# A frequency-domain filter and two gated layers on one core: the layout of the second block transposition

## The chip, the cores and the metric

The kernel runs on one core of a Trainium2 chip. The metric is the device time of one execution in microseconds; the time before is the median of three runs. The engines have short names here: PE is TensorE (matrix products, its weight loads are listed as PEld), DVE is VectorE, ACT is ScalarE, POOL is GpSimd, SP is SyncE, which only issues DMAs.

## The reference

Two sequences of 3008 tokens with 256 channels are filtered in the frequency domain, and the 6016 tokens then pass two layers of width 2048.

```python
X = np.fft.rfft(x, axis=1)                  # x: (2, 3008, 256)
F = (filt_r + 1j * filt_i)[None, :, :]      # (1505, 256)
y = np.fft.irfft(X * F, n=3008, axis=1)
h = y.reshape(6016, 256) @ moe_w_in         # (256, 2048)
g = np.where(h > 0, h, np.exp(np.minimum(h, 0)) - 1)
x1 = g @ moe_w_out                          # (2048, 256)
h = x1 @ moe2_w_in
g = h * np.clip(h + 3, 0, 6) / 6
out = g @ moe2_w_out
```

## The kernel before

The kernel has two parts. The first, up to about 141 us of the span, is the filter (the transform); the second, the other 1013 us, is the two layers, with matrix products in three passes each (lines 366 to 368 and 377). The change touches only the first part.

The length 3008 is 64 x 47, and each transform is a 47-point and a 64-point one in a row, forward and back, written as matrix products with constant matrices (`mats`). The work is cut into four blocks of 128 channels by one sequence (`ORDER`), and each block into 8 groups of 16 channels (`GD`): 32 rounds `i` in all (`NG`). In a round, PE runs `part_a` (line 309, 47-point forward), DVE's `turn_a` (line 545) transposes the result in blocks of 32 x 32 from PSUM to `spec`, PE runs `part_x` (line 317, 64-point forward), DVE multiplies by the filter in `products` (lines 552 and 554), PE runs `part_r` (lines 325 and 326, 64-point back), and DVE's `turn_r` (line 563) transposes that, again in blocks of 32 x 32, from PSUM to `back`. PE's loop runs `part_a(i + 2)`, `part_x(i + 1)`, `part_r(i)` in round `i`; DVE's runs `turn_a(i + 2)`, `products(i + 1)`, `turn_r(i)`. PSUM banks, `spec`, `prod_r` and `prod_i` are double.

`back` has two halves, one per block, each `[128, 32, 128]` fp32 in the order (time index `j`, channel `d`). Once all 8 groups of a block are in it, the last stage (47-point back) runs as `part_i(n)`, line 334: 7 pieces (`PIECES`) of up to 5 values of `j`. For each `j` the stationary operand is the 128 x 128 slice `back[:, half, j, :]`, 128 consecutive floats in each partition, and the moving operand is the constant `I1`, 94 columns. Every fp32 product is two instructions on PE and two weight loads, so a full piece is 10 loads and 10 matmuls, a block 64 of each, and all four blocks 256. The pieces of a block are spread over the first 7 of the next block's 8 rounds, one at the end of each (`piece_at`); those of the last block come after round 31.

ACT copies each piece to `ystage` (line 436) and SP stores it to `y0` (line 227). SP issues in a fixed order: in round `i` the filter values of round `i + 2` (`load_f`, line 219, three slots), in every second round more of `x` (line 212, four slots), then the store of the piece before. POOL multiplies the filter by a sign (line 616) and, every third round, adds up and rounds one of 8 sets of layer weights (lines 623 to 636); ACT has the rounding to `w_hi` (line 443) ahead of the copy of a piece in the same queue.

At the start PE runs 6 products on zeroed memory of `back` (line 340), for which DVE clears 512 floats per partition (line 565). After the last piece come two small products (line 360) and the first products of the layers (line 366).

Of the kernel before, what the change touches and what calls it, by code (L numbers as in the profile page):

```python
# [12 lines left out]
P = 128  # L13
# [7 lines left out]
Q, J, N2P = 2, 32, 48  # L21
AROWS = Q * N2P
GD = 16
# [3 lines left out]
ICOL = Q * N2  # L27
# [65 lines left out]
def build(nc, x_dev, f_dev, sign_dev, mats_dev, w_dev, out_dev):  # L93
    with ExitStack() as ctx:
        def sem(name):
            return ctx.enter_context(nc.semaphore(name))

        def sbuf(stack, name, shape, dt=F32):
            return stack.enter_context(nc.sbuf_tensor(name, shape, dt))
# [11 lines left out]
        with ExitStack() as fft:  # L111
            mats = sbuf(fft, "mats", [P, len(MATS) * P])
            sign = sbuf(fft, "sign", [P, K2])
            x_ring = sbuf(fft, "x_ring", [P, XSLOTS, 2 * GCOL])
            f_ring = sbuf(fft, "f_ring", [P, FSLOTS, 2, XCOL])
            spec = sbuf(fft, "spec", [P, 2, GCOL])
            prod_r = sbuf(fft, "prod_r", [P, 2, XCOL])
            prod_i = sbuf(fft, "prod_i", [P, 2, XCOL])
            back = sbuf(fft, "back", [P, 2, J, P])
        op_hi.append(sbuf(ctx, "op1_hi", [P, 7, T], F32R))  # L120
        op_lo.append(sbuf(ctx, "op1_lo", [P, 7, T], F32R))
        g_hi = sbuf(ctx, "g_hi", [P, 4, T], F32R)
# [4 lines left out]
        ps = ctx.enter_context(nc.psum_tensor("ps", [P, 8, 512], F32))  # L127

        def f32(ap):
            return ap.bitcast(F32)  # L130

        def mat(name):
            at = MATS.index(name) * P
            return mats[:, at:at + P]

        def ps_i(n):
            return ps[:, n % 2, 0:IJ * ICOL]

        def ps_a(i):
            return ps[:, 2 + i % 2, :]  # L140

        def ps_x(i):
            return ps[:, 4 + i % 2, 0:XCOL]

        def ps_r(i):
            return ps[:, 6 + i % 2, :].rearrange("p (d k) -> p d k", k=K2P)

        def bank(n):
            return ps[:, n, 0:T]
# [11 lines left out]
        zeroed = sem("zeroed")  # L161
        a_done, x_done, r_done, i_done = sem("a_done"), sem("x_done"), sem("r_done"), sem("i_done")
        spec_ready, prod_ready, back_ready = sem("spec_ready"), sem("prod_ready"), sem("back_ready")
# [25 lines left out]
        def piece_at(i):  # L189

            c, n = i // GROUPS - 1, i % GROUPS
            return c * PIECES + n if 0 <= c < len(ORDER) and n < PIECES else None

        def piece_cols(n):

            j0 = n % PIECES * IJ
            return n // PIECES, j0, min(IJ, J - j0)
# [102 lines left out]
        def _(pe):  # L300
# [27 lines left out]
            def part_i(n):  # L328
                pos, j0, nj = piece_cols(n)
                pe.wait_ge(back_ready, GROUPS * (pos + 1))  # L330
                if n >= 2:
                    pe.wait_ge(i_evac, n - 1)
                for j in range(nj):
                    last = pe.matmul(ps_i(n)[:, j * ICOL:j * ICOL + ICOL], back[:, pos % 2, j0 + j, :],
                                     mat("I1")[:, 0:ICOL], start=True, stop=True)
                last.then_inc(i_done, 1)

            pe.wait_ge(zeroed, 1)
            for _ in range(6):
                pe.matmul(ps[:, 0, :], back[:, 0, 0, :], back[:, 0, 0:4, :].rearrange("p j d -> p (j d)"),  # L340
                          start=True, stop=True)
            pe.wait_ge(a_mat_loaded, 16)
            part_a(0)
# [4 lines left out]
            for i in range(NG):  # L348
                if i + 2 < NG:
                    part_a(i + 2)  # L350
                if i + 1 < NG:
                    part_x(i + 1)
                part_r(i)
                n = piece_at(i)
                if n is not None:
                    part_i(n)
            for n in range(NPIECE - PIECES, NPIECE):
                part_i(n)
# [28 lines left out]
            for u in range(NU + 1):  # L387
                v = u - 1
                s, p = u // PAIRS, u % PAIRS
# [149 lines left out]
        @block.vector  # L539
        def _(dve):  # L540
            def turn_a(i):
                dve.wait_ge(a_done, i + 1)
                if i >= 2:
                    dve.wait_ge(x_done, i - 1)
                dve.transpose(spec[:, i % 2, :], ps_a(i)).then_inc(spec_ready, 1)

            def products(i):
                dve.wait_ge(x_done, i + 1)
                if i >= 2:
                    dve.wait_ge(r_done, i - 1)  # L550
                dve.wait_ge(f_loaded[i % FSLOTS], 16 * (i // FSLOTS + 1))
                dve.tensor_tensor(prod_r[:, i % 2, :], ps_x(i), f_ring[:, i % FSLOTS, 0, :], ALU.mult)
                dve.wait_ge(signed, i + 1)
                dve.tensor_tensor(prod_i[:, i % 2, :], ps_x(i), f_ring[:, i % FSLOTS, 1, :],
                                  ALU.mult).then_inc(prod_ready, 1)

            def turn_r(i):
                pos, g = i // GROUPS, i % GROUPS
                dve.wait_ge(r_done, i + 1)
                if pos >= 2 and g == 0:  # L560
                    dve.wait_ge(i_done, PIECES * (pos - 1))
                dst = back[:, pos % 2, :, g * GD:g * GD + GD].rearrange("p j d -> p d j")
                dve.transpose(dst, ps_r(i)).then_inc(back_ready, 1)

            dve.memset(back[:, 0, 0:4, :], 0.0).then_inc(zeroed, 1)
            for b in range(2):
                dve.memset(ps[:, 6 + b, :], 0.0).then_inc(zeroed, 1)
            turn_a(0)
            turn_a(1)
            products(0)  # L570
            for i in range(NG):
                if i + 2 < NG:
                    turn_a(i + 2)
                if i + 1 < NG:
                    products(i + 1)
                turn_r(i)

            def second_act(u, src, ap, clipped, ready, done):
                dve.wait_ge(ready, u + 1)
                if u < NS * PAIRS:  # L580
                    dve.tensor_scalar(ap, ap, 1.0, -1.0, ALU.min, ALU.add).then_inc(clipped, 1)  # L581
                    dve.wait_ge(clipped, u + 1)
                    dve.tensor_tensor(ap, src, ap, ALU.max).then_inc(done, 1)  # L583
                else:
                    dve.scalar_tensor_tensor(ap, ap, 6.0, src, ALU.min, ALU.mult).then_inc(done, 1)  # L585

            def low(tiles):
                return dve.tensor_tensor(g_lo[:, tiles, :], e[:, tiles, :], f32(g_hi[:, tiles, :]), ALU.subtract)  # L588

            for u in range(NU + 1):  # L590
                v = u - 1
                if v >= 0:
                    dve.wait_ge(hipair, v + 1)
                    low(slice(TILE21, TILE22 + 1)).then_inc(lopair, 1)
                    dve.wait_ge(hi12, v + 1)
                    low(TILE12).then_inc(lo12, 1)
                if u == NU:
                    break
                second_act(u, bank(BANK_B), e[:, TILE11, :], clip11, e11_ready, m11_done)
                dve.wait_ge(p5_done, u + 1)  # L600
                dve.wait_ge(s7_done, u + 1)
                dve.tensor_tensor(h2[:, 1, :], bank(BANK_C), s7[:], ALU.add).then_inc(h22_done, 1)  # L602
                dve.wait_ge(p4_done, u + 1)
                dve.tensor_tensor(h2[:, 0, :], bank(BANK_A), s7[:], ALU.add).then_inc(h21_done, 1)  # L604
                dve.wait_ge(hi11, u + 1)
                low(TILE11).then_inc(lo11, 1)
                second_act(u, h2[:], e[:, TILE21:TILE22 + 1, :], clippair, epair_ready, mpair_done)
                second_act(u, bank(BANK_C), e[:, TILE12, :], clip12, e12_ready, m12_done)
# [121 lines left out]
```

## Time and profile before

| | us |
|---|---|
| median of 3 runs | 1158.13 |
| lowest, highest | 1157.18, 1158.26 |
| the profiled execution, its own time | 1156.32 |
| its span, first to last instruction | 1154.5 |
| PE busy | 1128.6 (98% of the span) |
| DVE busy | 851.0 (74%) |
| ACT busy | 697.8 (60%) |
| POOL busy | 305.0 (26%) |

The granted TensorE clock is 0.998 of full speed over the whole span. A profile row names the line, engine and operation of a group of instructions. Matmuls are pipelined, and the ends in their records are modelled: how long one takes in a stream is read from the starts of two groups that follow each other, not from its duration. A row of the timeline merges neighbours of one line (x10 is ten instructions), and the brackets at its end give the idle time ahead of it and what ended that.

### The profile page before, as it was taken

What the parts mean: (1) busy time and instruction counts of PE and PEld (TensorE: products, weight loads), DVE (VectorE), ACT (ScalarE), POOL (GpSimd) and SP (SyncE); (2) the same over time, 40 slices, a digit from 0 to 9 for tenths busy, and PEclk for the clock granted to TensorE, in tenths of its full rate; (3) what the DMA queues carried; (4) which work ended last, traced back from release to release, by engine and by line L of the source; (5) the groups of instructions that cost most, each with busy time, mean ns of one, the idle gap of its engine ahead of it and who ended that gap; (6) DMA issues with size and microseconds to landing.
All of it is one profiled execution on the core that took longest, in us unless ns stands there. A gap on an engine that the chain in (4) does not pass through costs nothing.

```text
span 1154.5 us, 17183 instructions
## 1 busy us (share of the span) xinstructions
PE 1128.6 (98%) x6288; PEld 1069.8 (93%) x6288; DVE 851.0 (74%) x1347; ACT 697.8 (60%) x1293; POOL 305.0 (26%) x260
## 2 busy tenths in 40 slices
PE   9988999999999999999998899999999999999998
PEld 4655689999999999999998899999999999999998
DVE  6755488888888888887889877666766666666665
ACT  0211356666666666667666666666666666666665
POOL 4655523021211112120338742120302121111000
PEclk9999999999999999999999999999999999999999
DMA  8767400000010101000021200000000001010000
GB/s 254 226 212 216 151 24 28 28 28 28 1 55 1 54 1 49 6 27 28 28 82 55 91 1 28 27 28 27 28 28 28 28 9 46 1 55 1 28 1 28
DMA packets 33589, 59.52 MB, mean 52 GB/s; under 512 B 3456, under 2 KB 23552, under 8 KB 33504
## 3 DMA queue, kind: packets, MB, share of 16 engines
q1 hardware_dynamic: 33504, 58.42, 15.9%
q8 instruction: 50, 0.82, 0.3%
q14 instruction: 35, 0.29, 0.1%
HBM read 39.92 MB, written 18.48 MB: 51 GB/s over the span
## 4 chain that ended last, share of the span: by engine, by line
PE 83%; DVE 5%; POOL 4%; DMA 3%; ACT 2%; issue 2%; SPq 0%; ACTq 0%; DVEq 0%
PE ps L377 43%; PE ps L366 13%; PE ps L367 12%; PE ps L368 12%; DMA f_ring<-f_dev 3%; DVE e L583 2%; DVE e L581 1%; DVE g_lo L588 1%; POOL f_ring L616 1%; POOL w_lo L636 1%; POOL w_lo L634 1%; PE ps L340 1%; PE ps L309 1%; ACT w_hi L443 1%; ACT e L466 1%
## 5 line engine op out<-in xcount | busy, mean ns | idle before, releaser
L588 DVE TENSOR_TENSOR g_lo<-e,g_hi 128x376 fp32r<-128x376 f32 (+1 forms) x384 | 286.1, 773 | 113.5 <-ACT g_hi L494 113.1
L366 PE MATMUL ps<-op_hi,w_hi 128*128 128x376 f32 x896 | 300.4, 335 | 1.4 <-DVE h L602 1.4
L367 PE MATMUL ps<-op_hi,w_lo 128*128 128x376 f32 x896 | 299.7, 334 | 0.0
L368 PE MATMUL ps<-op_lo,w_hi 128*128 128x376 f32 x896 | 299.6, 334 | 0.0
L377 PE MATMUL ps<-g_hi,w_hi 128*128 128x376 f32 x1024 | 259.1, 334 | 7.1 <-ACT g_hi L494 7.1
L653 POOL TENSOR_TENSOR op_lo<-xr,op_hi 128x752 fp32r<-128x752 f32 x64 | 103.5, 1618 | 606.0 <-ACT op_hi L451 606.0
L377 PE MATMUL ps<-g_lo,w_hi 128*128 128x376 f32 x1024 | 259.3, 334 | 2.8 <-DVE g_lo L588 2.8
L377 PE MATMUL ps<-g_hi,w_lo 128*128 128x376 f32 x1024 | 259.8, 335 | 0.0
L377 PEld LDWEIGHTS ps<-g_hi,w_hi 128*128 128x128 f32 x1024 | 184.0, 188 | 9.1 <-ACT g_hi L494 9.0
L377 PEld LDWEIGHTS ps<-g_lo,w_hi 128*128 128x128 f32 x1024 | 184.1, 188 | 6.0 <-DVE g_lo L588 6.0
L377 PEld LDWEIGHTS ps<-g_hi,w_lo 128*128 128x128 f32 x1024 | 184.2, 188 | 0.0
L366 PEld LDWEIGHTS ps<-op_hi,w_hi 128*128 128x128 f32 x896 | 168.7, 188 | 4.6 <-DVE h L602 3.7
L367 PEld LDWEIGHTS ps<-op_hi,w_lo 128*128 128x128 f32 x896 | 168.7, 188 | 0.1
L368 PEld LDWEIGHTS ps<-op_lo,w_hi 128*128 128x128 f32 x896 | 168.5, 188 | 0.0
L581 DVE TENSOR_SCALAR e<-e 128x376 f32<-128x376 f32 (+1 forms) x192 | 94.8, 494 | 52.5 <-ACT e L466 52.1
L489 ACT COPY ps<-ps 128x376 f32<-128x376 f32 x128 | 58.9, 460 | 112.3 <-PE ps L368 112.3
L494 ACT CAST g_hi<-e 128x752 fp32r<-128x752 f32 x128 | 105.3, 823 | 16.7 <-DVE e L583 15.3
L518 ACT CAST g_hi<-e 128x376 fp32r<-128x376 f32 x128 | 64.9, 507 | 80.6 <-DVE e L583 53.8
L602 DVE TENSOR_TENSOR h<-ps,s 128x376 f32<-128x376 f32 x128 | 70.2, 549 | 32.6 <-PE ps L368 28.0
L468 ACT ACTIVATE e<-h 128x752 f32<-128x752 f32 x64 | 53.3, 833 | 62.5 <-DVE h L604 62.5
L585 DVE SCALAR_TENSOR_TENSOR e<-e,ps 128x376 f32<-128x376 f32 x128 | 69.3, 541 | 24.9 <-ACT e L468 24.1
L585 DVE SCALAR_TENSOR_TENSOR e<-e,h 128x752 f32<-128x752 f32 x64 | 64.6, 1009 | 20.2 <-ACT e L468 20.0
(50 smaller groups left out, 1216.5 us busy)
## 6 DMA issues: line engine op xcount, KB each, us to landing
f_ring<-f_dev SPq DMA_DIRECT2D x32, 384.0 KB, 4.8
xr<-y SPq DMA_DIRECT2D x64, 188.0 KB, 3.0
w_raw<-w_dev SPq DMA_DIRECT2D x32, 256.0 KB, 3.8
y<-ystage SPq DMA_DIRECT2D x16, 376.0 KB, 2.5
out_dev<-ystage SPq DMA_DIRECT2D x16, 376.0 KB, 2.5
x_ring<-x_dev SPq DMA_DIRECT2D x15, 384.0 KB, 5.7
y<-ystage SPq DMA_DIRECT2D x24, 235.0 KB, 2.7
x_ring<-x_dev SPq DMA_DIRECT2D x2, 192.0 KB, 3.5
```

Of the source, the lines that this page charges most:

```text
L366: pe.matmul(out, w_hi[:, p, cols], hi, start=start, stop=False, skip_group_check=True)
L367: pe.matmul(out, w_lo[:, p, cols], hi, start=False, stop=False, skip_group_check=True)
L368: pe.matmul(out, w_hi[:, p, cols], lo, start=False, stop=True, skip_group_check=True).then_inc(done, 1)
L377: last = pe.matmul(out_bank(o, t), w[:, p, at:at + P], g[:, tile, :], start=first, stop=final, skip_group_check=True)
L489: act.copy(bank(BANK_B), bank(BANK_A)).then_inc(copy1_done, 1)
L494: act.copy(g_hi[:, TILE21:TILE22 + 1, :], e[:, TILE21:TILE22 + 1, :]).then_inc(hipair, 1)
L518: act.copy(g_hi[:, TILE11, :], e[:, TILE11, :]).then_inc(hi11, 1)
L581: dve.tensor_scalar(ap, ap, 1.0, -1.0, ALU.min, ALU.add).then_inc(clipped, 1)
L585: dve.scalar_tensor_tensor(ap, ap, 6.0, src, ALU.min, ALU.mult).then_inc(done, 1)
L588: return dve.tensor_tensor(g_lo[:, tiles, :], e[:, tiles, :], f32(g_hi[:, tiles, :]), ALU.subtract)
L602: dve.tensor_tensor(h2[:, 1, :], bank(BANK_C), s7[:], ALU.add).then_inc(h22_done, 1)
L653: pool.tensor_tensor(op_lo[s % 2][:, lo:hi, :], xr[:, 1 + lo:1 + hi, :], f32(op_hi[s % 2][:, lo:hi, :]), ALU.subtract).then_inc(op_lo_done, 1)
```

## The change

`back` gets the order (channel `d`, time index `j`) instead of (`j`, `d`). The result of `turn_r` is then one run of 512 consecutive floats per partition, as that of `turn_a` is; before, its 32 values of one `d` lay 512 bytes apart. `part_i` reads for each `j` the slice `back[:, half, :, j]`: 128 floats per partition that lie 32 floats, 128 bytes, apart; before, they lay one beside the other. The cleared memory and the products at the start are written for the new order and have the sizes of before: 512 consecutive floats, 128 of which are the stationary operand. No instruction is added, dropped or moved on any engine, and the waits are those of before.

```diff
--- before.py
+++ after.py
@@ -116,7 +116,7 @@
             spec = sbuf(fft, "spec", [P, 2, GCOL])
             prod_r = sbuf(fft, "prod_r", [P, 2, XCOL])
             prod_i = sbuf(fft, "prod_i", [P, 2, XCOL])
-            back = sbuf(fft, "back", [P, 2, J, P])
+            back = sbuf(fft, "back", [P, 2, P, J])
         op_hi.append(sbuf(ctx, "op1_hi", [P, 7, T], F32R))
         op_lo.append(sbuf(ctx, "op1_lo", [P, 7, T], F32R))
         g_hi = sbuf(ctx, "g_hi", [P, 4, T], F32R)
@@ -331,13 +331,14 @@
                 if n >= 2:
                     pe.wait_ge(i_evac, n - 1)
                 for j in range(nj):
-                    last = pe.matmul(ps_i(n)[:, j * ICOL:j * ICOL + ICOL], back[:, pos % 2, j0 + j, :],
+                    last = pe.matmul(ps_i(n)[:, j * ICOL:j * ICOL + ICOL], back[:, pos % 2, :, j0 + j],
                                      mat("I1")[:, 0:ICOL], start=True, stop=True)
                 last.then_inc(i_done, 1)
 
             pe.wait_ge(zeroed, 1)
             for _ in range(6):
-                pe.matmul(ps[:, 0, :], back[:, 0, 0, :], back[:, 0, 0:4, :].rearrange("p j d -> p (j d)"),
+                pe.matmul(ps[:, 0, :], back[:, 0, 0:4, :].rearrange("p d j -> p (d j)"),
+                          back[:, 0, 0:16, :].rearrange("p d j -> p (d j)"),
                           start=True, stop=True)
             pe.wait_ge(a_mat_loaded, 16)
             part_a(0)
@@ -559,10 +560,10 @@
                 dve.wait_ge(r_done, i + 1)
                 if pos >= 2 and g == 0:
                     dve.wait_ge(i_done, PIECES * (pos - 1))
-                dst = back[:, pos % 2, :, g * GD:g * GD + GD].rearrange("p j d -> p d j")
-                dve.transpose(dst, ps_r(i)).then_inc(back_ready, 1)
-
-            dve.memset(back[:, 0, 0:4, :], 0.0).then_inc(zeroed, 1)
+                dst = back[:, pos % 2, g * GD:g * GD + GD, :].rearrange("p d j -> p (d j)")
+                dve.transpose(dst, ps[:, 6 + i % 2, :]).then_inc(back_ready, 1)
+
+            dve.memset(back[:, 0, 0:16, :], 0.0).then_inc(zeroed, 1)
             for b in range(2):
                 dve.memset(ps[:, 6 + b, :], 0.0).then_inc(zeroed, 1)
             turn_a(0)
```

## Rows read from the trace of the kernel before

**Rows 1.** The page, busy time and share of the span by engine, whole kernel
```profile
PE 1128.6 (98%) x6288; PEld 1069.8 (93%) x6288; DVE 851.0 (74%) x1347; ACT 697.8 (60%) x1293; POOL 305.0 (26%) x260
```

**Rows 2.** Groups by line and shape, 0 to 240 us: count | busy, mean ns | idle before
```profile
L563 DVE STREAM_TRANSPOSE back<-ps 128x512 f32<-128x512 f32 x32 | 34.1, 1066 | 5.2 <-PE ps L326 5.2
...
L334 PE MATMUL ps<-mats,back 128*128 128x94 f32 x256 | 32.2, 274 | 4.4 <-ACT ystage L436 3.3 <-DVE back L563 1.1
L334 PEld LDWEIGHTS ps<-mats,back 128*128 128x128 f32 x256 | 32.0, 191 | 11.5 <-issue 4.6 <-DVE back L563 1.8
...
L545 DVE STREAM_TRANSPOSE spec<-ps 128x512 f32<-128x512 f32 x32 | 22.0, 688 | 18.3 <-PE ps L309 18.0
```

**Rows 3.** Timeline, 19 to 25 us, TensorE: start us, us, what, count
```profile
19.29 0.81 PE L325 MATMUL ps<-prod_r,mats 128*128 128x384 f32 x2
...
21.44 0.81 PE L317 MATMUL ps<-spec,mats 128*128 128x384 f32 x2
22.08 0.81 PE L325 MATMUL ps<-prod_r,mats 128*128 128x384 f32 x2
```

**Rows 4.** Timeline, 19 to 25 us, VectorE: in brackets idle before, releaser
```profile
17.98 1.06 DVE L563 STREAM_TRANSPOSE back<-ps 128x512 f32<-128x512 f32 x1 [0.27 <-PE ps L326]
18.91 0.66 DVE L545 STREAM_TRANSPOSE spec<-ps 128x512 f32<-128x512 f32 x1
...
20.78 1.07 DVE L563 STREAM_TRANSPOSE back<-ps 128x512 f32<-128x512 f32 x1 [0.27 <-PE ps L326]
```

**Rows 5.** Timeline, 31 to 57 us, TensorE, rounds with a piece of the last stage
```profile
36.07 0.81 PE L325 MATMUL ps<-prod_r,mats 128*128 128x384 f32 x2
...
39.98 0.81 PE L325 MATMUL ps<-prod_r,mats 128*128 128x384 f32 x2
...
49.09 1.25 PE L334 MATMUL ps<-mats,back 128*128 128x94 f32 x10
50.18 1.05 PE L309 MATMUL ps<-x_ring,mats 96*128 96x512 f32 x2
```

**Rows 6.** Line 334 by stretches: busy us (instructions) of PE and PEld, clock, DMA
```profile
36.00:65.00 29.00, 8.07 (x64) 8.25 (x64) 1.00 0.61 199
65.00:120.00 55.00, 13.22 (x104) 13.18 (x104) 1.00 0.72 226
120.00:132.00 12.00, 3.08 (x24) 3.15 (x24) 1.00 0.32 103
```

**Rows 7.** TensorE by stretches: busy us (instructions), granted clock, DMA
```profile
36.00:66.00 30.00, 30.00 (x131) 1.00 0.62 202
66.00:120.00 54.00, 46.06 (x197) 1.00 0.71 226
```

**Rows 8.** Timeline, 57 to 132 us, TensorE: first products' matmuls of four rounds
```profile
65.58 0.81 PE L325 MATMUL ps<-prod_r,mats 128*128 128x384 f32 x2
...
71.29 0.91 PE L325 MATMUL ps<-prod_r,mats 128*128 128x384 f32 x2 [1.64 <-DVE prod_i L554]
...
121.23 0.81 PE L325 MATMUL ps<-prod_r,mats 128*128 128x384 f32 x2
...
129.90 0.84 PE L325 MATMUL ps<-prod_r,mats 128*128 128x384 f32 x2
```

**Rows 9.** Chain that ended last, 50 to 70 us: start us, us, what
```profile
51.05 4.36 DMA f_ring<-f_dev
...
63.79 0.77 ACT ystage L436 x2
...
64.73 4.86 DMA f_ring<-f_dev
```

**Rows 10.** Chain that ended last, 128 to 143 us
```profile
131.42 1.05 DVE back L563
...
132.52 1.37 PE ps L334 x10
...
139.89 0.65 PE ps L334 x4
140.54 1.29 PE ps L360 x4
```

## The prediction

> **What bounds the kernel now.** The page comes first: PE is busy for 98% of the span, DVE for 74% [rows 1]. The diff touches only the first 141 us of 1154.5, so the whole span says little, and the groups of that stretch come next [rows 2]. Two facts stand there. The second block transposition (line 563) takes 1066 ns, the first one (line 545) 688 ns, for the same 128 x 512 from PSUM to SBUF. The last stage (line 334) has 256 weight loads.
>
> Then the timeline, to see who waits. In rounds without a piece of the last stage PE starts line 325 every 2.79 us [rows 3], with its groups one straight behind the other: 0.64 us for two matmuls of 384 columns, 0.84 ns a column. DVE waits 0.27 us for PE before each second transposition [rows 4]. So here PE sets the pace, but barely. In rounds with a full piece the round is 3.91 us, from line 325 to line 325 [rows 5]. The 10 matmuls of a piece take 1.09 us up to the next line's start, 109 ns each [rows 5]. By columns, 94 x 0.84 ns would be 79 ns. What spaces them is therefore more likely the weight load: 128 columns in 109 ns, 0.85 ns each, the rate of the moving operand.
>
> From 36 to 66 us PE is busy for 30.00 of 30.00 us. From 66 to 120 us it is busy for 46.06 of 54 [rows 7]. The chain that ended last shows what holds it there: the filter values are requested at 51.05 and again at 64.73 us, and between the two lie their landing, POOL's sums and roundings and the copy of two pieces by ACT at 63.79 [rows 9]. That loop takes 13.7 us for three rounds and holds no transposition. After 120 us PE sets the pace again. At the end of the part the last second transposition (131.42) releases the last block's 64 loads, which run from 132.52 until the next line's products start at 140.54 [rows 10].
>
> **The change part by part.** *The second transposition, 32 times.* It now writes 512 consecutive floats, exactly what the first does. In the steady rounds that is 0.66 us in place of 1.07 [rows 4], so 0.41 us less, 13 us of DVE in all. Nearly all of it lies beside PE's work: in the rounds up to 66 us PE is back to back and DVE waits for it, so DVE only waits longer; from 66 to 120 us DVE waits for DMA and POOL. It is exposed once, at 131.42 us, where the last piece waits for it: **-0.4 us**.
>
> *The strided weight loads, 256 times.* The trace has no stationary operand with a stride, so the price is bounded. Below zero is excluded: 128 columns are still loaded, now at 0.85 ns each. Zero is the lower end, and a weak row speaks for it: line 317 reads 24 of every 32 floats and takes 0.64 us [rows 3], as line 325 does, which reads consecutive ones. But its breaks come every 24 floats, not at every float. The nearest row for a break at each float is the transposition: 0.41 us for 512 elements is 0.80 ns an element. It is a write by another engine, at 512 bytes, but of the same memory and at a step beyond which no two elements lie together. For 128 elements that makes 102 ns more. I take **0.102 us a load**, so 0.211 in place of 0.109. As the upper end I take twice this, since a read may have to wait for its data where a write does not.
>
> [rows 4] show that a stride in this memory costs about what an element costs. The Trainium skill, Advanced Engine Details and Errata, SBUF Cachelines, says that full speed wants accesses that hit the same 16-byte line, and that a different line at each access has a penalty; at 128 bytes each float has its own line. It states no size of the penalty; by it the price is above zero.
>
> What lies on the path, stretch by stretch, with the loads counted in [rows 6]:
>
> - Up to the round that starts line 325 at 65.58 us: 64 loads, PE back to back. 64 x 0.102 = 6.5 us, all exposed. That round now starts at 72.1.
> - From 65.58 to 121.23 us [rows 8] there are 12 rounds and 104 loads in 55.65 us. PE alone would need 12 x 2.80 + 104 x 0.109 = 44.9, so it holds 10.7 us of waits, such as the 1.64 us at 71.29. The windows show 7.9 us of them idle; the rest is in the modelled ends and in loads that wait. With dear loads PE alone needs 33.6 + 104 x 0.211 = 55.5 us, the length that the stretch has already. The 10.6 us added disappear in the waits, and the lag stays 6.5 - 0.1 = 6.4. This holds only if POOL's and SP's loop isn't itself pushed back. It needs the copy of a piece at 63.79 [rows 9]. That is PE's sixth piece, two rounds of 3.91 us behind the one at 49.09 [rows 5]: it ends at 58.0 us now, and 60 dear loads later (6.1 us) at 64.1. So the loop is pushed by 0.3 us there, and further on it has more room.
> - From 121.23 to 129.90 us [rows 8]: 24 loads and no waits to speak of. 24 x 0.102 = 2.4 us. Lag at the last round: 8.8.
> - The last block: 8.0 us now for 64 loads [rows 10], of which 64 x 0.109 = 7.0 are loads and 1.0 is a wait for `ystage`. It becomes 64 x 0.211 = 13.5; the stores then have time. +5.5 us.
>
> *The cleared memory and the first six products*: same sizes, consecutive; 0. *The layers*: untouched, they start later; 0. The instruction order is that of before.
>
> Sum: 8.8 + 5.5 - 0.4 = **+13.9 us**. The profiled execution took 1156.3, so 1170.2. The median of the runs lies 1.8 above it (1158.1): **1172.0**.
>
> **The rivals.**
>
> *B: the stride is free for a load.* Mechanism: PE asks for one float of each partition only every 0.85 ns, and what the transposition shows is a cost of writing, or of DVE's access, not of the memory. For it speaks line 317. Against it speaks that nothing in that row breaks at each float. Then only the -0.4 is left: 1155.9 for the profiled one, **1157.7** for the median. This is the case on the other side of slower, and the point that decides is the price of a load: the waits from 66 to 120 us take up to 10.7 us over 192 loads (0.056 us each), and a price of 0.056 would leave 0.0 at the last round, 64 x 0.056 - 1.0 = 2.6 at the end, minus 0.4: 2.2 us, or 0.2%. Below about 165 ns a load the change can't be told from none; at 211 it is slower.
>
> [rows 5] show 109 ns for a load of 128 consecutive columns. The Trainium skill, TensorE: Matmul & The Clock Gate, LDWEIGHTS, gives the time of a load as the number of columns by 1.2 GHz, 107 ns, and has no term for a stride; the trace agrees for consecutive columns. By this rule the outcome is B.
>
> *C: faster by over 0.2%.* DVE's 13 us would have to count. Place: from 66 to 120 us, where DVE runs late rounds after a DMA wait, the second transposition stands ahead of the next first one in its queue. If it were last there in six rounds, free loads and 0.41 us each would give 0.4 + 2.5: **1155.2**. Against it: the chain of that stretch holds no line 563, and DVE's waits there end with DMA and POOL.
>
> *D: a load pays much more.* At 0.204 us over, twice the price: 64 x 0.204 = 13.1; then 33.6 + 104 x 0.313 = 66.2 against 55.65, +10.5; 24 x 0.204 = 4.9; the end 64 x 0.313 - 8.0 = 12.0; minus 0.4. That is +40.1: **1198**. It decides as soon as the loads take more than all waits can hold, which is at 0.103 each.
>
> **How the numbers follow.** A, the forecast, gets 0.55, with a range of its own from 1166 (0.07 us a load) to 1178 (PE's waits only half used). B gets 0.32, from 1156 to 1159.5, and holds the prices too small to be seen. C gets 0.05, D 0.08. About 0.2%, 2.3 us, is what a measurement of this kernel can tell from no change. A range that leaves out no more than 2 in 10 must hold A and B: 1156.0 to 1178.0, 0.87 with both whole. Faster 0.05, same 0.32, slower 0.63 (A and D).
>
> **What would show it.** Second transposition: the line's mean falls from 1066 to about 688 ns, and DVE's wait for line 326 grows from 0.27 to about 0.6 us in the first rounds; this holds in A and B. The loads: the start of line 309 behind a full piece comes 2.1 us after the start of line 334 in A, 1.09 in B, 3.1 in D. Rounds with a full piece are 4.9 us in A and 3.9 in B. PE's idle time from 66 to 120 us is nearly gone in A. Line 360, behind the last piece, starts near 154.4 us in A and 140.1 in B; from there on both traces are alike. Rounds without a piece stay at 2.79 us in all cases; were they shorter, DVE had been the bound there. The forecast is wrong if the loads in the piece keep 109 ns, if the price lies under 0.056, or if PE's lag pushes the loop of DMA, POOL and ACT so that waits and dear loads add up (then up to 1182).

## The result and the profile after

| | before | changed |
|---|---|---|
| median, us | 1158.2 (4 runs) | 1172.1 (4 runs) |
| lowest, highest, us | 1157.2, 1158.3 | 1171.0, 1172.8 |
| the profiled execution, us | 1156.32 | 1172.80 |
| its span, us | 1154.5 | 1170.9 |

The ratio is 1.012, with a 95% interval from 1.0104 to 1.0136: the change makes the kernel 1.2% slower. The forecast was 1172.0.

Busy time on the page of the changed kernel (its lines after the diff are one higher), to be read beside [rows 1]:

```profile
PE 1155.5 (99%) x6288; PEld 1101.9 (94%) x6288; DVE 843.4 (72%) x1347; ACT 698.8 (60%) x1293; POOL 305.3 (26%) x260
```

DVE lost 7.6 us of work, PE's busy time grew by 26.9. The groups by line and shape, up to 160 us, beside [rows 2] (count | busy, mean ns | idle before):

```profile
L334 PEld LDWEIGHTS ps<-mats,back 128*128 128x128 f32 x256 | 59.2, 309 | 4.8 <-DVE back L564 1.4
L334 PE MATMUL ps<-mats,back 128*128 128x94 f32 x256 | 56.7, 379 | 0.8 <-DVE back L564 0.8
...
L564 DVE STREAM_TRANSPOSE back<-ps 128x512 f32<-128x512 f32 x32 | 22.9, 716 | 9.3 <-PE ps L326 9.3
L546 DVE STREAM_TRANSPOSE spec<-ps 128x512 f32<-128x512 f32 x32 | 22.9, 716 | 49.2 <-PE ps L309 47.6
```

A load of the last stage is on record for 309 ns in place of 191, and both transpositions have the same mean, 716 ns. How long a load really takes is in the starts of the timeline, beside [rows 5, 8]: a piece, then three rounds that answer to 65.58, 121.23 and 129.90 before:

```profile
47.34 2.21 PE L334 MATMUL ps<-mats,back 128*128 128x94 f32 x10
49.39 1.05 PE L309 MATMUL ps<-x_ring,mats 96*128 96x512 f32 x2
...
71.89 0.81 PE L325 MATMUL ps<-prod_r,mats 128*128 128x384 f32 x2
...
126.97 0.81 PE L325 MATMUL ps<-prod_r,mats 128*128 128x384 f32 x2
...
137.87 0.84 PE L325 MATMUL ps<-prod_r,mats 128*128 128x384 f32 x2
```

The piece takes 2.05 us up to the next line, where it took 1.09. The three rounds come 6.31, 5.74 and 7.97 us later than before; 0.23 of it was there already ahead of the first piece (line 325 at 36.30 for 36.07). That is scatter of the start and not the change: in the traces shown here and below, of kernels with either order, the first piece starts anywhere from 36.48 to 37.66 us. A round without a piece still takes 2.79 us, one with a full piece 4.88 in place of 3.91. PE by stretches, beside [rows 7] with 46.06 of 54 us:

```profile
66.00:120.00 54.00, 54.00 (x196) 1.00 0.69 206
```

No wait is left. The end of the part, in the chain that ended last, beside [rows 10]:

```profile
139.40 0.73 DVE back L564
...
140.17 14.29 PE ps L334 x64
154.46 2.57 PE ps L361 x4
...
158.51 0.44 PE ps L367
```

Line 361 (360 before) starts 13.92 us later than before; the forecast of the change in the total was 13.9. But it takes 2.57 us in place of 1.29. The windows of all engines show why: busy us (instructions) of PE, PEld, DVE, ACT, POOL, then the granted clock, DMA share and GB/s:

```profile
142.00:144.00 2.00, 2.00 (x11) 2.00 (x10) 0.00 (x0) 0.55 (x1) 0.00 (x0) 1.00 0.00 0
144.00:146.00 2.00, 2.00 (x11) 2.00 (x10) 0.00 (x0) 0.55 (x1) 0.00 (x0) 0.55 0.32 120
146.00:150.00 4.00, 4.00 (x20) 4.00 (x20) 0.00 (x0) 1.10 (x2) 0.00 (x0) 0.50 0.33 122
...
154.00:156.00 2.00, 2.00 (x6) 1.32 (x5) 0.00 (x0) 0.49 (x2) 0.00 (x0) 0.50 0.47 161
156.00:158.00 2.00, 2.00 (x7) 1.52 (x6) 0.00 (x0) 0.00 (x1) 0.00 (x0) 0.54 0.78 225
158.00:160.00 2.00, 1.95 (x10) 1.32 (x9) 0.00 (x0) 1.55 (x4) 0.05 (x1) 1.00 0.53 168
```

The granted clock falls from 1.00 to 0.50, from 2.4 to 1.2 GHz, within the window from 144 to 146 us, in the last block's 64 dear loads, and is back from 158. Before, it was 1.00 in all of this.

The layers give part of that back, and lose something of their own later. The same instruction of the layers, well behind the filter, first before, then in the changed kernel:

```profile
175.07 0.33 PE L367 MATMUL ps<-op_hi,w_lo 128*128 128x376 f32 x1
189.79 0.33 PE L368 MATMUL ps<-op_hi,w_lo 128*128 128x376 f32 x1
```

It comes 14.72 us later, and that distance holds up to about 610 us. Between 610 and 680 us it grows to 16.49. There the clock fell three times more in the changed kernel's profiled execution, for some 3.4 us each (the windows give 0.53 from 629 to 632.5 us, 0.55 from 649 to 652.5 and 0.53 from 670 to 673.5), and once in that of the kernel before (0.60 from 614 to 618). Other kernels below have none to two such falls in this place, so this part is scatter of single executions.

### The profile page after: what moved, and what is told of

It reads as the page before. It is cut to its first block, busy times and chain, and to the rows that moved or that the text cites. A ratio compares the mean times of both kernels' runs of the same rounds, so it can differ in the third digit from the quotient of the medians.

```text
span 1170.9 us, 17183 instructions
## 1 busy us (share of the span) xinstructions
PE 1155.5 (99%) x6288; PEld 1101.9 (94%) x6288; DVE 843.4 (72%) x1347; ACT 698.8 (60%) x1293; POOL 305.3 (26%) x260
## 4 chain that ended last, share of the span: by engine, by line
PE 94%; DVE 4%; ACT 1%; issue 1%; ACTq 0%
PE ps L378 43%; PE ps L367 13%; PE ps L369 13%; PE ps L368 13%; PE ps L334 5%; PE ps L309 2%; PE ps L317 2%; PE ps L325 2%; PE ps L326 2%; DVE e L584 2%; DVE e L582 1%; PE ps L340 1%; DVE g_lo L589 1%; ACT e L467 1%; PE ps L361 0%
```

## Experiments

The kernel before was measured again beside three groups of the experiments: its medians were 1156.4 us (beside experiment 1 and the steps of 8 and 16 bytes), 1158.8 (experiment 3, the wide operand and 12 bytes) and 1157.7 (the last block, the pairs and 124 bytes), its single runs 1154.5 to 1162.9. A total is therefore compared by ratio and interval with the kernel before of its group, and what is under 2 us is read from the traces.

**1. Which half of the change costs.** The layout of the changed kernel, with consecutive loads:

```diff
-back[:, pos % 2, :, j0 + j],
+back[:, pos % 2, 4 * (j0 + j):4 * (j0 + j) + 4, :].rearrange("p d j -> p (d j)"),
```

> Half of the change alone: the second transposition writes its 512 consecutive floats as in the changed kernel, but each load of the last stage takes 128 consecutive floats of the block, in the old access pattern and so not the right values. Theory (the loads carry all of the loss, DVE's time is hidden): transposition 0.72 us, piece spacing 1.09 us, PE idle from 66 to 120 us as before (7.9 us), and a gain of 0.3 to 0.4 us at the last transposition only, 1157.8. Rival (DVE's 11 us matter in the stretch in which PE waits): waits of line 325 for line 554 shrink, 1155.5 or less. Rival (the loss comes from the transposition colliding with another access when it runs at full speed): 1160 or more.

1157.1 us for 1156.4 before, ratio 1.0004, interval 0.9995 to 1.0014. The group of the second transposition and PE's wait for DVE between 36 and 131 us (total, times, longest):

```profile
L564 DVE STREAM_TRANSPOSE back<-ps 128x512 f32<-128x512 f32 x32 | 22.7, 710 | 4.1 <-PE ps L326 3.9
...
PE ps L325 <- DVE prod_i L555: 6.1, 5, 2.2
```

PE by stretches (busy us, instructions, clock, DMA):

```profile
66.00:120.00 54.00, 46.17 (x191) 0.97 0.75 226
```

The transposition is as quick as in the changed kernel, the kernel is as slow as before, and PE's wait for line 555 did not shrink (6.1 us; 4.7 before over the same stretch; this execution had the clock at 0.50 for some 3 us near 82 us, which the wait may hold in part). DVE's 11 us are hidden, and a quick transposition does no harm by itself. The -0.3 at the last transposition is too small for the interval; the trace has it, as PE's wait of 0.81 us ahead of the last block in place of 1.14.

The other half alone, the layout of before with loads at a step of 128 bytes:

```diff
+flat = back[:, pos % 2].rearrange("p j d -> p (j d)")
-back[:, pos % 2, j0 + j, :],
+flat[:, j0 + j:j0 + j + 4065:32],
```

> The other half alone: the second transposition writes as before, 1.07 us, and each load takes 128 floats of the block that lie 128 bytes apart, as in the changed kernel (other values than the right ones). Theory (the loads carry all of the loss): piece spacing 2.04 us, PE without idle time from 66 to 128 us, half clock at the end of the part, 1172.1 + 0.35 for the slower last transposition = 1172.5. Rival (the loss needs both halves): 1165 or less.

1169.9 us, ratio 1.0117, interval 1.0102 to 1.0133, the changed kernel's 1.012 again. (The 1172.5 expected was counted from a slower sample of the kernel before; the difference to the 1156.4 measured beside it is 13.6 us.) Its groups:

```profile
L335 PEld LDWEIGHTS ps<-mats,back 128*128 128x128 f32 x256 | 59.2, 309 | 5.1 <-DVE back L564 1.8
...
L564 DVE STREAM_TRANSPOSE back<-ps 128x512 f32<-128x512 f32 x32 | 34.9, 1092 | 9.2 <-PE ps L326 9.2
```

309 ns a load, as in the changed kernel, beside a transposition of 1092. PE has no idle time from 66 to 120 us here either, and the clock falls to 0.50 in the last block. The loss is that of the loads alone.

**2. What a load pays for.** The same edit with other steps, one run each (none of these four computes the reference):

> The kernel before with loads of 128 floats that lie 8 bytes apart, two to a 16-byte line (other values than the right ones). Theory 1 (each load element pays when it comes from another 16-byte line than the last, unless two share it): free, piece spacing 1.09 us, about 1158. Theory 2 (any step above one float costs): spacing above 1.3 us, up to 2.04 us and 1172. Theory 3 (cost grows with the distance): 1.1 to 1.2 us.

> The kernel before with loads of 128 floats that lie 16 bytes apart, one to a line (other values than the right ones). Theory 1 (lines of 16 bytes): full price, piece spacing 2.04 us, 1172. Theory 3 (cost grows with the distance, full at 128 bytes): spacing clearly under 2.04 us, 1.2 to 1.5. Theory 4 (only a large power of two costs): free, 1.09 us.

> The kernel before with loads of 128 floats that lie 12 bytes apart (other values than the right ones). Three neighbours in four come from another 16-byte line. If each change of line costs the same, about 0.1 us, unless hidden by the free slot that a second hit gives: three quarters of the price, piece spacing 1.8 us. If the line is fetched in the time of two elements, 128 x 3/4 fetches at 1.6 ns = 154 ns a load: spacing 1.55 us. If only steps of 16 bytes and more cost: 1.15 us.

> The kernel before with loads of 128 floats that lie 124 bytes apart, each in another line, at no power of two (other values than the right ones). Theory (another 16-byte line at each float is all that counts): piece spacing 2.04 to 2.17 us, as at 128 and 16 bytes, 1170 to 1175. Rival (part of the price comes from the distance being a power of two): clearly less, 1.5 us or under.

One piece and the line behind it in each timeline. A step of 8 bytes:

```profile
49.52 1.31 PE L335 MATMUL ps<-mats,back 128*128 128x94 f32 x10
50.66 1.05 PE L309 MATMUL ps<-x_ring,mats 96*128 96x512 f32 x2
```

12 bytes:

```profile
49.92 1.81 PE L335 MATMUL ps<-mats,back 128*128 128x94 f32 x10
51.58 1.05 PE L309 MATMUL ps<-x_ring,mats 96*128 96x512 f32 x2
```

16 bytes:

```profile
47.66 2.34 PE L335 MATMUL ps<-mats,back 128*128 128x94 f32 x10
49.84 1.05 PE L309 MATMUL ps<-x_ring,mats 96*128 96x512 f32 x2
```

124 bytes:

```profile
47.43 2.32 PE L335 MATMUL ps<-mats,back 128*128 128x94 f32 x10
49.58 1.05 PE L309 MATMUL ps<-x_ring,mats 96*128 96x512 f32 x2
```

The last block's pieces follow one another without a round between, so the starts of ACT's copies there show ten whole loads. Before, and at 12 bytes:

```profile
133.91 0.55 ACT L436 COPY ystage<-ps 128x470 f32<-128x470 f32 x1 [3.09 <-PE ps L334]
135.03 0.55 ACT L436 COPY ystage<-ps 128x470 f32<-128x470 f32 x1 [0.56 <-PE ps L334]
```

```profile
143.98 0.55 ACT L437 COPY ystage<-ps 128x470 f32<-128x470 f32 x1 [1.58 <-PE ps L335]
146.12 0.55 ACT L437 COPY ystage<-ps 128x470 f32<-128x470 f32 x1 [1.58 <-PE ps L335]
```

| step, bytes | stretches of 16 bytes (lines) per load | piece between rounds, us | ten loads in the last block, us (clock there) | single run, us |
|---|---|---|---|---|
| 4 (before) | 32 | 1.09 | 1.12 (1.00) | - |
| 8 | 64 | 1.14 | 1.19 (1.00) | 1158.2 |
| 12 | 96 | 1.66 | 2.13 (0.50) | 1167.2 |
| 16 | 128 | 2.18 | 2.33 (0.50) | 1175.1 |
| 124 | 128 | 2.15 | 2.30 (0.50) | 1175.0 |
| 128 (changed) | 128 | 2.05 | 2.18 (0.50) | 1172.1 (median) |

Each piece between rounds is nine such loads and one product of 94 columns (0.08 us): 9 x 0.112 + 0.08 = 1.09 before, 9 x 0.218 + 0.08 = 2.04 at 128 bytes. The first load of the ten is not seen, as it runs beside the product ahead of it.

The distance doesn't count beyond 16 bytes, and a power of two isn't dear (128 bytes is even the cheapest of the last three, for which no run gives a reason). A load of 8 bytes' step is nearly free, one of 12 lies half way. One reading comes near all but that last row: a load takes a line in about 1.8 ns, the time of two of its columns. By it 32 lines are hidden behind the 112 ns of the columns, 64 lines take 115 ns, 96 take 173 and 128 take 230. With nine loads to a piece the measured ones are 118, 176 (1.66 less 0.08, by nine) and 233. It is a fit to these six steps and not shown beyond them. The form of it that stood in the expectation gave 1.55 for 12 bytes, and 1.66 was measured, against 1.8 and 1.15 for the others. The Trainium skill, Advanced Engine Details and Errata, SBUF Cachelines, has the rule that two hits on a 16-byte line absorb the latency and one does not. The runs at 8 and 16 bytes agree.

**3. Where the waits of 66 to 120 us went.** The forecast let 10.7 us of waits swallow the dear loads there. The waits were put down to a loop through ACT, whose copy of a piece stands behind a rounding of weights that waits for POOL. So the copy was moved ahead of it, in the kernel before:

```diff
 for i in range(NG + PIECES):
-    for p in range(PAIRS):
-        if i == w_step(p):
-            weight_hi(p)
     n = piece_at(i - 1) if i <= NG else None
     if n is not None:
         evac_piece(n)
+    for p in range(PAIRS):
+        if i == w_step(p):
+            weight_hi(p)
```

> The kernel before, with ACT copying the piece of the round before ahead of the rounding to w_hi (and not behind it); it computes the whole reference. Theory (the waits of 66 to 120 us come from a loop that runs through ACT's copy standing behind the rounding, so that SP's store and the next request of filter values wait for POOL): the loop is open, PE waits there for at most 2 of 7.9 us, 1148 to 1152 where the kernel before has 1156.4. Rival (POOL's own work, or the DMA engines, set the 13.7 us for three rounds): 1155 to 1157, PE still idle for 6 us or more.

1146.1 us against 1158.8, ratio 0.9888, interval 0.9865 to 0.991. PE from 66 to 120 us, and the chain that ended last in the stretch of [rows 9]:

```profile
66.00:120.00 54.00, 53.89 (x243) 1.00 0.75 231
```

```profile
53.17 1.08 PE ps L334 x10
54.26 0.89 PE ps L309 x2
```

PE is busy for 53.89 of 54 us, and the chain runs on PE, where it ran through DMA and POOL. The cause of the waits is shown, and this kernel is faster than both. It gained more than the 1148 to 1152 us expected: line 360 starts at 130.26 us for 140.38, so 10.1 us were to be had and not only the 7.9 that the windows show idle. The same exchange in the changed kernel:

> The same exchange in the changed kernel; it computes the whole reference. Theory (with dear loads PE sets the pace throughout and has no wait left that the loop causes): nothing, within 0.5 us of the changed kernel, so 13 to 14 us above the kernel before. Rival (the loop still costs the changed kernel something): 2 us or more less than the changed kernel.

1171.6 us (1170.5 to 1172.0), the changed kernel's time; PE from 66 to 120 us:

```profile
66.00:120.00 54.00, 54.00 (x196) 1.00 0.70 205
```

It had no wait to give back. Between these two kernels, both nearly without waits in that stretch, little hides the loads: 1171.6 - 1146.1 = 25.5 us. That is nearly twice the 13.9 of the change itself; the loop's waits had paid for the rest.

**4. The clock.**

> The changed kernel with the constant moving operand of the last stage taken 128 columns wide in place of 94 (the others are zeros, and the next product overwrites them); it computes the whole reference. Theory 1 (the load sets the spacing, and a matmul has 204 ns to fill): piece spacing stays 2.04 us. Theory 2 on the clock (it fell to half in the last block because the loads leave the array idle for 125 of 204 ns, and busier products keep it up): no half clock at 145 to 158 us, line 361 for 1.3 us in place of 2.6, total 2 to 3 us under the changed kernel. Rival on the clock (any row of products spaced by such loads loses it): clock 0.57 from 142 to 158 us as before, no gain.

```diff
-last = pe.matmul(ps_i(n)[:, j * ICOL:j * ICOL + ICOL], back[:, pos % 2, :, j0 + j],
-                 mat("I1")[:, 0:ICOL], start=True, stop=True)
+last = pe.matmul(ps[:, n % 2, j * ICOL:j * ICOL + P], back[:, pos % 2, :, j0 + j],
+                 mat("I1"), start=True, stop=True)
```

1169.9 us (1169.1 to 1171.0), 1.7 under the 1171.6 of the changed kernel with the exchange, measured beside it, and 2.2 under the changed kernel. The single runs overlap (that kernel had 1170.5 to 1172.0), so the trace decides. PE at the end of the part, and the chain there:

```profile
142.00:158.00 16.00, 15.94 (x73) 1.00 0.38 127
```

```profile
139.76 14.34 PE ps L334 x64
154.10 1.27 PE ps L361 x4
```

With 128 columns in the same spacing the clock stays at 1.00, where it was 0.57 over the same window, and line 361 takes 1.27 us. The other traces agree. In all six kernels whose last block has 94 columns and loads at 12 bytes or more (the changed one, with and without the exchange, and the steps of 12, 16, 124 and 128 bytes in the order of before) the clock fell to 0.50 in that row. In none of those with loads at 4 or 8 bytes, nor in this one, did it fall there.

The gain in the total is not all from there. The instruction of the layers that comes at 189.79 us in the changed kernel comes at 189.13 here and at 189.33 in the changed kernel with the exchange, so behind the filter this kernel leads by 0.7 and 0.2 us only. The rest arises between 610 and 680 us, where this profiled execution has no fall of the clock. What half clock in the last block costs a whole run is therefore well under 1 us, not the 2 to 3 expected.

The last block's 64 loads take 14.3 us here too. ACT's copies show the spacing of its pieces, here

```profile
144.46 0.55 ACT L437 COPY ystage<-ps 128x470 f32<-128x470 f32 x1 [1.65 <-PE ps L334]
146.66 0.55 ACT L437 COPY ystage<-ps 128x470 f32<-128x470 f32 x1 [1.65 <-PE ps L334]
```

and in the changed kernel at half clock

```profile
144.90 0.55 ACT L437 COPY ystage<-ps 128x470 f32<-128x470 f32 x1 [1.72 <-PE ps L334]
147.09 0.55 ACT L437 COPY ystage<-ps 128x470 f32<-128x470 f32 x1 [1.64 <-PE ps L334]
```

2.20 and 2.19 us for 10 loads: at a step of 128 bytes half clock doesn't slow the loads, only the products behind them. It does at 12 bytes, where ten loads take 2.13 us at half clock (lines in experiment 2) and 1.76 by the pieces at full clock. The two would fit together if half clock slowed a load's columns only: 213 ns for 128 columns is 1.7 ns each, about twice the 0.85 of before, and the loads at 128 bytes, with 219 ns at full clock, are above that already. This is argued; no run has consecutive loads at half clock to test it.

> The changed kernel, but the last block keeps the old layout and consecutive loads (its values are misplaced). Theory (half clock comes from 64 dear loads in a row with nothing beside them, and the loads cost 0.096 us each): the last block takes 8.0 us again, no half clock, so only the lag of PE up to round 31 is left, 8.0 us: 8 us above the kernel before, 6 under the changed one. Rival (the clock falls for the dear loads of the rounds before, which take 2.04 of every 4.9 us): half clock stays and the gain is 4 us at most.

```diff
+block = back[:, pos % 2, :, j0 + j]
+if pos == len(ORDER) - 1:
+    block = back[:, pos % 2, 4 * (j0 + j):4 * (j0 + j) + 4, :].rearrange("p d j -> p (d j)")
-back[:, pos % 2, :, j0 + j],
+block,
```

with `turn_r` writing the old layout for that block. The expectation errs in one point: writing and reading agree here, and the kernel computes the whole reference. 1164.8 us, ratio 1.0063, interval 1.0047 to 1.008: 7.1 above the kernel before, measured beside it, and 7.3 under the changed kernel. In the trace the products behind the last block start at 148.37 us for 140.38, the 8.0 us expected. PE at the end:

```profile
142.00:158.00 16.00, 15.09 (x97) 1.00 0.44 146
```

No half clock, although the rounds before have the dear loads as ever. In this kernel the fall belongs to the last block's row of them.

**5. A layout between the two,** on top of the exchange of experiment 3:

```diff
-back = sbuf(fft, "back", [P, 2, J, P])
+back = sbuf(fft, "back", [P, 2, J // 2, P, 2])
-back[:, pos % 2, j0 + j, :],
+back[:, pos % 2, (j0 + j) // 2, :, (j0 + j) % 2],
-dst = back[:, pos % 2, :, g * GD:g * GD + GD].rearrange("p j d -> p d j")
-dve.transpose(dst, ps_r(i)).then_inc(back_ready, 1)
+dst = back[:, pos % 2, :, g * GD:g * GD + GD, :].rearrange("p j d e -> p d j e")
+dve.transpose(dst, ps_r(i).rearrange("p d (j e) -> p d j e", e=2)).then_inc(back_ready, 1)
```

> A layout between the two, with two time indices j side by side for each channel, in the kernel whose ACT copies the piece first: the transposition writes runs of 8 bytes, the loads take floats 8 bytes apart; it computes the whole reference. Theory (both sides are nearly free when two floats share a line): transposition 0.75 us or less in place of 1.07, piece spacing 1.15 us, so -0.3 at the last transposition, +0.006 x 256 = 1.5 for the loads: 1147.3 where the exchange alone gave 1146.1. Rival (DVE holds PE up in places there, since it waits only 5.6 us in all): 1145 or less. Rival (runs of 8 bytes still cost a write its full price): 1.07 us, 1147.6.

1147.1 us (1147.0 to 1147.4), ratio 0.9913, interval 0.9898 to 0.9928. Its groups:

```profile
L334 PEld LDWEIGHTS ps<-mats,back 128*128 128x128 f32 x256 | 33.7, 196 | 7.0 <-DVE back L564 1.4 <-issue 0.2
...
L564 DVE STREAM_TRANSPOSE back<-ps 128x512 f32<-128x512 f32 x32 | 22.9, 714 | 6.2 <-PE ps L326 6.1
```

Both sides are quick at once, 714 ns and 196 ns. It gives nothing here, since only PE's side is paid for and that has the 5 ns a load. Whether it costs anything beside the exchange alone is not shown. The intervals overlap, and line 361 starts at 130.42 us for 130.26; most of the 1.2 us between the two profiled executions arises from 640 to 650 us, where the clock was 0.83 in this one and 1.00 in the other. That 1147.3 was forecast is luck. In a kernel that DVE bounds, this layout would be the one to try; no run here is of such a kernel.

## Why the prediction was right, and where it wasn't

**The mechanism** held up to the end of the filter: the load spaces the last stage, the strided load is dearer, DVE's gain is hidden, and of the loads' price a part disappears in waits. Behind that the forecast had both traces alike, and they aren't (the clock, below).

**The price of a load**, taken as 0.102 us from the transposition: it is 0.107 in a row (219 against 112 ns), and 0.096 by the ten of a piece between rounds (2.05 for 1.09), of which only nine show. That it came so near is luck in part. The 0.41 us that it was taken from held a record of line 545 that was too short, as the next paragraph but one says. By the means, 1066 against 716 ns, the transposition's surcharge is 0.35 us, 0.68 ns an element, and the same working would have given 0.088. That both surcharges come from a new line at each float is argued and not shown: both all but vanish for floats in pairs (714 ns and 1.14 us), but the steps between were tried on the loads alone.

**The lag by stretches**, forecast 6.5, 6.4 and 8.8 us, was 6.1, 5.5 and 7.7, without the 0.23 of the start. At 0.096 the same working gives 6.1, 5.4 and 7.7: only the price was off. One side sum of the forecast is wrong: at a price of 0.056 the lag at the last round would not be 0.0, since the 24 loads behind 121.23 us lie past the waits and add 1.3, so 3.5 us in all and not 2.2. That waits and dear loads would not add up was the bold step; PE without idle time, and the exchange that did nothing in the changed kernel, show it.

**The last transposition** gave 0.32 us for 0.41 (0.73 in place of 1.05 in the chain). The steady rounds of the changed kernel show 0.72 us for either transposition:

```profile
18.22 0.72 DVE L564 STREAM_TRANSPOSE back<-ps 128x512 f32<-128x512 f32 x1 [0.27 <-PE ps L326]
19.08 0.72 DVE L546 STREAM_TRANSPOSE spec<-ps 128x512 f32<-128x512 f32 x1
...
21.01 0.72 DVE L564 STREAM_TRANSPOSE back<-ps 128x512 f32<-128x512 f32 x1 [0.27 <-PE ps L326]
```

The 0.66 us of line 545 before was too short: its record starts at 18.91 us, while that of line 563 ahead of it runs to 19.04 [rows 4]. And DVE's wait for line 326 did not grow to 0.6 us in the first rounds as forecast, it stayed 0.27. DVE waits ahead of the next instruction instead, the first transposition: from 18.94 to 19.08 us in these rows, and over the stretch the idle time that ends with line 309 grew from 18.0 to 47.6 us, that with line 326 from 5.2 to 9.3. The line's mean, 716 ns for the forecast 688, says what the steady rows did not.

**The last block**: forecast 13.5 us, 14.1 measured from its first start to line 361's (140.17 to 154.25 by the timeline), against 7.9 before: +6.2 for +5.5, through the 219 ns. The forecast had 211 ns, and 109 before with 1.0 us of waits for `ystage`; at 112 ns before, 0.7 us are left for waits.

**What the sum left out** lies behind the filter, the clock first. Line 361 and the first products behind it take 1.7 us more up to the third group of products (4.26 us after 154.25; 2.52 after 140.38 before; 2.49 with wider products). In all, at that point: 0.23 + 7.74 - 0.32 + 6.22 + 1.74 = 15.6, as the trace has it (158.51 for 142.90). The layers take 0.9 of it back up to 175 us, where the distance is 14.72. Without the scatter of the start that is 14.5, so the sum of 13.9 is 0.6 too small. It holds two errors of opposite sign, the price between rounds (1.1 too much) and the last block (0.7 too little), and beside them 0.85 us that arise behind the filter (14.72 less the 13.87 at line 361). The kernel with wide products, its clock at 1.00, has 0.5 of these too (13.56 at line 361, 14.06 in the layers), for which no run gives the cause. That leaves some 0.35 us for the clock.

The profiled execution was forecast at 1170.2 and took 1172.8. The two profiled executions are 16.5 us apart, 14.7 by the above and 1.8 that arise between 610 and 680 us, together with the falls of the clock there. The medians are 13.9 apart, and the interval of the ratio leaves room for 12.0 to 15.8. So the hit of 0.1 us is luck: nothing here can tell 13.9 from 14.7. That the change costs 12 to 16 us, and by which terms, is what was foreseen.

The two kernels of experiment 3 make the cleaner test of the loads, since little hides them: 192 loads x 0.096 = 18.4, 6.2 for the last block, less 0.3, together 24.3. In the traces the products behind the last block lie 23.6 us apart (153.83 for 130.26) and those of the layers 24.4 (189.33 for 164.97), and 25.5 us separate the medians.

**The rivals.** B (loads free) is refuted by the read-only half; it is nearly true at a step of 8 bytes. Line 317's row, 24 consecutive floats and a gap, says nothing on single floats. C (DVE's time counts) is refuted by the write-only half. D's price was not reached by any step.

## What to carry to other kernels

When a layout can be right for the writer or for the reader, price both by what they touch per element, and pay on the engine that waits: here DVE's 11 us were free and 256 loads of PE were not. Two floats side by side are enough for both. Waits on the pacing engine can hide a loss (about 10 us here) as well as show where a gain is to be had: moving one copy ahead of a waiting instruction in ACT's queue was worth 1.1%, about as much as the change under study cost.

## What was not expected of the hardware

- A stationary operand at a step of 8 bytes loads at nearly full speed (1.14 for 1.09 us a piece), at 12 bytes it takes half the surcharge (1.66), and from 16 bytes on all of it (2.05 to 2.18).
- The granted clock fell to 0.50 while PE was on record as busy all the time: 64 matmuls of 94 columns, each spaced 219 ns by its load. With 128 columns at the same spacing it stayed at 1.00. The loads at 128 bytes took no longer at half clock (2.19 us for ten, 2.20 at full clock), those at 12 bytes did (2.13, and 1.76 at full clock).
- Half clock in the last block and the first products behind it made these products 1.7 us longer, and 0.9 of the lag at that point was gone again in the first 20 us of the layers. Between 610 and 680 us single executions have none to three falls of some 3.4 us each. The three kernels without any there (the quick transposition alone, the exchange alone, the wide products) kept their distance to the kernel before within 0.1 us, the one with three lost 1.8 us.
- In the transposition from PSUM a destination in runs of 8 bytes is as quick as a consecutive one (714 and 716 ns), single floats 512 bytes apart take 1066.
